# Visit places, two early banks, weights ahead of alpha and later query copies in a two-stage attention and MLP kernel

## The reference, cut to what matters

```
state = alpha[t][:, None] * state + outer(k[t], v[t])     # 4 batches, 8 heads, 768 tokens, 48 channels
y[t]  = q[t] @ state
x     = y, arranged as 3072 tokens x 384
h = x @ w_in  (384 x 2048);   g = h * sigmoid(1.702 h);   x = g @ w_out  (2048 x 384)
h = x @ w_in2 (384 x 2048);   g = h - tanh(h);            out = g @ w_out2 (2048 x 384)
```

## Time and profile before

| what | value |
|---|---|
| median of 3 executions | 976.02 us (975.45 to 976.64) |
| the profiled execution's own time | 975.9 us |
| its span | 974.1 us |
| TensorE busy | 951.4 us, 98% of the span |
| VectorE busy | 548.1 us, 56%, but 7 to 9 tenths in the first 18 of 40 slices |
| ScalarE / GpSimd busy | 334.1 us / 283.0 us |
| DMA | 59.07 MB; full in 26 to 40 us and in 44 to 50 us |

### The profile page before, as it was taken

How to read it: one execution, slowest core, us unless ns; L and a number is a source line. 1 busy time by engine, 2 the same in 40 slices (tenths; PEclk the granted TensorE clock), 3 DMA queues, 4 the chain that set the end, 5 groups by cost and what they waited for, 6 DMA issues and landing times.

```text
span 974.1 us, 22270 instructions
## 1 busy us (share of the span) xinstructions
PE 951.4 (98%) x9364; PEld 823.0 (84%) x9364; DVE 548.1 (56%) x1348; ACT 334.1 (34%) x683; POOL 283.0 (29%) x314
## 2 busy tenths in 40 slices
PE   5899999999999999999999999999999999999998
PEld 5789999999999988888888888888888888888886
DVE  7879997878888877776221223334334343343332
ACT  2342333332332332333234554333333333333332
POOL 2565655556556554444001542000000000000000
PEclk9999999999999999999999999999999999999999
DMA  7933232423323432321103332020020010200000
GB/s 156 262 82 88 56 86 48 112 51 80 84 61 62 115 64 47 103 50 22 36 38 126 96 96 74 0 65 1 1 66 1 24 41 1 65 1 1 33 1 33
DMA packets 136533, 59.07 MB, mean 61 GB/s; under 512 B 114288, under 2 KB 131824, under 8 KB 136432
## 3 DMA queue, kind: packets, MB, share of 16 engines
q1 hardware_dynamic: 133616, 55.54, 22.8%
q10 hardware_dynamic: 2816, 2.10, 0.7%
HBM read 43.45 MB, written 14.16 MB: 59 GB/s over the span
## 4 chain that ended last, share of the span: by engine, by line
PE 91%; DVE 3%; DMA 3%; SPq 1%; POOL 1%; issue 1%; ACT 1%; ACTq 0%; DVEq 0%; POOLq 0%
PE pX L760 38%; PE pZ L784 26%; PE pX L784 14%; PE pX L624 2%; PE pZ L719 2%; PE pZ L652 2%; PE pZ L610 1%; PE pZ L662 1%; DMA k<-k_t 1%; PE pX L755 1%; PE pX L638 1%; DVE scores L1065 1%; PE pZ L710 1%; SPq L323 1%; DVE w_lo L1071 1%; POOL r L518 1%
## 5 line engine op out<-in xcount | busy, mean ns | idle before, releaser
L760 PE MATMUL pX<-x_hi,w_hi 128*128 128x512 f32 (+2 forms) x624 | 227.9, 365 | 0.7 <-ACT g L913 0.7
L760 PE MATMUL pX<-x_hi,w_lo 128*128 128x512 f32 (+2 forms) x624 | 227.5, 365 | 0.0
L760 PE MATMUL pX<-x_lo,w_hi 128*128 128x512 f32 (+2 forms) x624 | 227.5, 365 | 0.0
L1081 DVE TENSOR_TENSOR g_lo<-g,g_hi 128x512 fp32r<-128x512 f32 (+2 forms) x208 | 133.3, 641 | 155.0 <-ACT g_hi L922 154.8
L1179 DVE TENSOR_TENSOR g<-pX,sg 128x512 f32<-128x512 f32 x96 | 66.3, 691 | 177.7 <-ACT sg L915 177.7
L784 PE MATMUL pZ<-g_hi,w_hi 128*128 128x512 f32 (+2 forms) x414 | 151.0, 365 | 0.0
L784 PE MATMUL pZ<-g_lo,w_hi 128*128 128x512 f32 (+2 forms) x414 | 150.9, 365 | 0.0
L784 PE MATMUL pZ<-g_hi,w_lo 128*128 128x512 f32 (+2 forms) x414 | 150.9, 364 | 0.0
L922 ACT ACTIVATE g_hi<-g 128x512 fp32r<-128x512 f32 (+2 forms) x208 | 121.3, 583 | 78.0 <-DVE g L1179 74.5
L913 ACT ACTIVATE g<-pX 128x512 f32<-128x512 f32 (+3 forms) x144 | 65.7, 456 | 212.6 <-PE pX L760 175.8
L760 PEld LDWEIGHTS pX<-x_hi,w_hi 128*128 128x128 f32 x624 | 117.6, 188 | 17.8 <-ACT g L913 1.1
(11 more groups left out here) (100 smaller groups left out, 1137.4 us busy)
## 6 DMA issues: line engine op xcount, KB each, us to landing
v<-v_l SPq DMA_DIRECT2D x96, 48.0 KB, 2.6
x_raw<-hidden SPq DMA_DIRECT2D x6, 768.0 KB, 5.8
attn_out<-y SPq DMA_DIRECT2D x94, 48.0 KB, 1.9
out_t<-o SPq DMA_DIRECT2D x10, 384.0 KB, 3.4
alpha<-a_t SPq DMA_DIRECT2D x24, 128.0 KB, 3.0
r<-q_t SPq DMA_DIRECT2D x24, 128.0 KB, 3.0
k<-k_t SPq DMA_DIRECT2D x24, 128.0 KB, 3.0
w_raw<-w_in SPq DMA_DIRECT2D x16, 192.0 KB, 2.4
```

The lines of the kernel that those rows point to most:

```text
L760: last = nc.tensor.matmul(pH(N)[:, 0:w], win(wp, f, m), XS[T % 2][xp][:, m, 0:w], start=(n == 0), stop=(n == len(terms) - 1))
L1081: nc.vector.tensor_tensor(GL[:, columns(N)], g_raw(N), GH[:, columns(N)].bitcast(F32), ALU.subtract).then_inc(gl_done, 1)
```

## The change

Four edits. The visits of items 3 to 16 move: item 3 from N = 4 to 6, 4 from 8 to 10, 5 from 12 to 14, 6 from 16 to 18, 7 from 20 to 22, 8 stays at 25, 9 goes from 30 to 32, 10 from 33 to 35, 11 from 36 to 38, 12 from 39 to 41, 13 from 42 to 44, 14 from 45 to 47, 15 from 49 to 50, 16 from 52 to 53; from item 17 (N = 55) on all are the same. up(1) and up(3) go into the bank O0 in place of H0, so that up(N) for N up to 4 waits for one activation less, while down(0) waits for the fourth activation and for the states of items 0 and 1. SP issues weight group 3 ahead of alpha of unit 3. The plain query copies stand one N later as long as the visit is in block 0 or 1 (with the moved visits: at N = 6, 14, 22, 31 in place of 3, 11, 19, 29, then 37 and 43 in place of 35 and 41, 49 in place of 48, and the same from there on). `x_at` is not changed.

```diff
-    starts = ([0, 4, 8, 12, 16, 20, 25, 30] + [33 + 3 * n for n in range(5)] + [49 + 3 * n for n in range(5)]
+    starts = ([0, 6, 10, 14, 18, 22, 25] + [32 + 3 * n for n in range(8)] + [55 + 3 * n for n in range(3)]
               + [64 + 2 * n for n in range(29)])
...
         def pH(N):
+            if N in (1, 3):
+                return O0
             return H0 if N < L1B * NF or N % 2 == 0 else H1
...
                 if U == 1:
                     load_w(sp, 2)
+                    load_w(sp, 3)
                 if U + 2 < UNITS:
                     load_alpha(U + 2)
-                if U == 1:
-                    load_w(sp, 3)
...
                 if N < L1N:
-                    if N:
-                        pe.wait_ge(g_done, N)
+                    if N > 1:
+                        pe.wait_ge(g_done, N if N > 4 else N - 1)
...
                 if T < PLAIN:
-                    pe.wait_ge(g_done, N + 1)
+                    pe.wait_ge(g_done, max(4, N + 1))
...
+                if N == 0:
+                    pe.wait_ge(state_step, states_before(LEAD))
                 for m in range(KC):
...
-            queries_at = {VISIT_OF[j + 1] - 1: j // 2 + 1 for j in range(LEAD, ITEMS - 2, 2)}
+            queries_at = {VISIT_OF[j + 1] - (VISIT_OF[j + 1] >= L1P): j // 2 + 1 for j in range(LEAD, ITEMS - 2, 2)}
...
-                    nc.scalar.activation(g_raw(N), H0[:, 0:width(T)], ACT.Gelu_apprx_sigmoid).then_inc(g_done, 1)
+                    nc.scalar.activation(g_raw(N), pH(N)[:, 0:width(T)], ACT.Gelu_apprx_sigmoid).then_inc(g_done, 1)
```

## The result

The changed kernel takes 985.43 us (median of 4, 984.14 to 986.89) against 975.74 us before: ratio 1.0092, 95% interval 1.0077 to 1.0107. It is slower by 9.7 us; I had forecast slower by 3.6. The profiled execution's span is 985.1 us against 974.1; at 986.9 us it is the slowest of the four.

A forecast was written before the change was run, and what follows sets the result against it. TensorE was taken as the bound, with VectorE's list setting block 2's earliest start. From 975.9 us: -1.1 balance from up(32), +1.7 low clock, +2.2 wait at block 3, +0.8 its clock = 979.5; range 975.8 to 982.2.

The forecast's parts named there:

- The step of block 3's input: At up(44): TensorE waits a new 2.2 us, since ScalarE's x_hi waits for the input load; bounds 1.2 and 3.
- Its clock: Low clock behind the wait at up(44): 0.8 us taken, bounds 0 and 1.7.
- The clock behind up(32): Low clock expected after 4.5 us of idle TensorE at up(32): 1.7 us, bounds 0 and twice that.
- Seven items in front of block 2: VectorE's list ahead of block 2 is unchanged, 29.1 us behind item 6's scores; x_lo ends at 92.7, bounds 91.3 and 95.
- The balance from up(32) on: 3.4 us gained by an earlier up(32), 2.83 given back for visit 9, 0.6 gained at visits 10 and 11: net gain 1.1.
- TensorE gains 2.5 us: Ahead of visit 3: early ups fit four more products (2.68 us) in for 0.14, so TensorE gains 2.5 us.
- The weights: Group 3 ahead of alpha of unit 3: alpha lands about 46.8 (bounds 43.0 and 49.5), so visit 5 waits 1.4 us.
- VectorE does not hold block 2: Faster rival: x_lo of block 2 could end at 86.7 in step with TensorE; 972.4 us, chance 0.13.
- the clock holds: No-change rival: the waits come without low clock; 977.0 us, or 975.8 with alpha landing as early as now; chance 0.15.
- The weights cost more: Slower rival: alpha of unit 3 at 49.5, x_lo at 94.5, both waits with full 1.7 us low clock; 982.2 us, chance 0.12.
- The copies still hold the keys: Rival: ScalarE's query copy of unit 3 still delays the keys; same time as the forecast, counted within its 0.60.
- The first rival: The case of x_lo of block 2 ending at 86.7 in step with TensorE; 972.4 us, chance 0.13.

The follow-up runs named there:

- v_visits: Kernel before with only the visits moved, plus the wait on the states of items 0 and 1 ahead of down(0); 985.1 us, ratio 1.0086.
- a_nobanks: Changed kernel without the early banks (up(1) and up(3) again into H0; the wait on the states stays); 985.84 us.
- a_noweights: Changed kernel with weight group 3 again issued behind alpha of unit 3; 985.46 us.
- a_xhigh44: Changed kernel with x_hi and x_lo of block 3 at N = 44 in place of 42; 980.4 us, ratio 1.0054 to the kernel before.
- v_late: Kernel before with only the later visits moved (item 9 at N = 32 and on every third slice, items 3 to 8 unmoved); 983.12 us, ratio 1.0078.
- a_fixed: Changed kernel with w_out remainders behind x_lo of block 2 and x_hi and x_lo of block 3 at N = 44; 973.45 us, ratio 0.9988.
- v_queries: Kernel before with only the later query copies; 974.35 us, ratio 0.9982.
- c_querieswlox13: Kernel before with later query copies, w_out remainders behind x_lo of block 2, and block 4's x_hi and x_lo at N = 61; 976.94 us, ratio 1.0020.
- v_banks: Kernel before with only the early banks (O0 for up(1) and up(3), with the waits that go with it); 974.48 us, ratio 0.9979.
- a_fixed_now: Changed kernel with late w_out remainders, block 3's x_hi and x_lo at N = 44, and weight group 3 again behind alpha; 974.19 us, ratio 0.9997.

## Why the prediction was wrong

**Direction and places right.** Slower, by the two waits I had named at up(32) and up(44), with the wait in visit 5 gone. The step of block 3's input had 2.2 us (bounds 1.2 and 3) and measured 2.4, with 2.9 between the visits; ScalarE waits for the input as described, behind the activation of slice 42:

```profile
139.26 0.84 ACT L876 ACTIVATE x_hi<-x_raw 128x768 fp32r<-128x768 f32 x1 [3.60 <-DMA x_raw<-attn_out]
```

Its clock, for which I took 0.8 between 0 and 1.7, is 1.0. The clock behind up(32) was put at 1.7 and is 1.9, by what is left over in the account above. That both terms come out so near is partly luck: the stretch behind up(32) is 6.8 us long and not 3.4 as in the trace that I took the price from, and the wait at up(44) is 3.1 to 3.4 us in v_visits, a_nobanks and a_noweights, above my bound of 3.

**What failed is the step "Seven items in front of block 2": the end of `x_lo`.** I took 92.7, with an upper bound of 95; it ended at 98.6, so up(32) came 5.9 us later than forecast, and the forecast misses by the same (979.5 against 985.4). The balance from up(32) on had 3.4 us gained from an `x_lo` earlier than before; there was no such gain, but 2.5 us of loss. VectorE in the changed kernel:

```profile
48.53 0.29 DVE L964 TENSOR_TENSOR sf<-alpha 112x128 f32<-112x128 f32 x1 [2.06 <-DMA alpha<-a_t]
...
66.85 0.42 DVE L1050 TENSOR_TENSOR scores<-pX,mask 128x256 f32<-128x256 f32 x1 [0.96 <-PE pX L639]
...
82.25 1.26 DVE L964 TENSOR_TENSOR t<-f 112x32 f32<-112x32 f32 x1
83.55 1.18 DVE L964 TENSOR_TENSOR f<-t 112x16 f32<-112x16 f32 x1
84.64 0.17 DVE L961 COPY f<-t 112x16 f32<-112x16 f32 x1
84.76 0.19 DVE L964 TENSOR_TENSOR f<-f,t 112x16 f32<-112x16 f32 x1
84.86 0.70 DVE L964 TENSOR_TENSOR t<-f 112x8 f32<-112x8 f32 x1
...
97.62 0.96 DVE L1080 TENSOR_TENSOR x_lo<-x_raw,x_hi 128x768 fp32r<-128x768 f32 x1
```

Two halves. First, item 6's scores started at 66.85 and not at 63.6, since TensorE was late: "TensorE gains 2.5 us" at visit 3 was wrong. I had costed the early ups by their waits alone. They ran 0.67 apart, and then TensorE stood still for 3.2 us with 3.4 us at a granted clock of 0.50 behind it, some 1.7 us of time; visit 3 began at 39.90 and not 35.1. Second, from item 6's scores to the end of `x_lo` are 31.7 us and not 29.1. The work is the same, as I said; the durations are not. The four product steps and the copy that took 0.17 to 0.19 us each before (80.54 to 81.17 for all) took from 82.25 to 85.48 here, 1.26, 1.18 and 0.70 for three of them. Visit 7 had moved from N = 20 to 22 and visit 8 stayed at 25, so visit 8 now begins 6.9 us behind it (9.6 before), and GpSimd's multiplications, which wait for visit 8's products, fall beside VectorE's steps for the next unit. Before, and then after:

```profile
80.54 0.19 DVE L961 TENSOR_TENSOR t<-f 112x32 f32<-112x32 f32 x1
80.77 0.19 DVE L961 TENSOR_TENSOR f<-t 112x16 f32<-112x16 f32 x1
```
```profile
82.15 1.31 POOL L534 TENSOR_TENSOR k<-k,sf 112x512 f32<-112x512 f32 x1 [2.15 <-PE pX L639]
83.42 5.56 POOL L519 TENSOR_TENSOR r<-r,alpha 112x512 f32<-112x512 f32 x5
```

Each of the three long steps starts about 0.1 us behind a GpSimd multiplication and ends within 0.05 us of that one's end (83.46, 84.68 and 85.53); the copy of the same size stays at 0.17, and one step, at 84.76, stays at 0.19. The Trainium skill, "SBUF — State Buffer", section "Who interferes with whom", says that VectorE and GpSimd share one pair of ports under an exclusive lock, and that a VectorE instruction with two SBUF inputs contends with a GpSimd instruction that reads SBUF. The trace agrees: three of the four operations with two inputs stretch and the copy does not. v_visits has the same pattern (1.31 and 1.22 us at 81 and 82 us) without the gap of 31 us. That the overlap is the cause is read from the traces; I did not move GpSimd's work to prove it.

Of the two, the second is what v_visits, a_nobanks, a_noweights and a_xhigh44 share with the changed kernel. In a_noweights item 6's scores start at 64.4, nearly where I had them, and `x_lo` still ends 31.1 us later, at 95.4. The gap is not shared: a_nobanks has none and is as slow. The size of the first half is also one of this execution: a_xhigh44, the same code up to block 3's input, has a gap of 0.8 us, waits 3.2 us for scores ahead of visit 5 instead, and ends `x_lo` at 100.5. Nor is the overlap the loss against the kernel before. `x_lo` ends at 95.4 to 96.8 in v_visits, a_nobanks and a_noweights and at 96.07 in the kernel before, and v_late, without long steps, is slow as well. What costs is that visit 9 was taken out of the very stretch in which TensorE then has nothing to do; I had set against it a gain at `x_lo` that did not come.

**The weights.** Alpha of unit 3 landed about 48.5, where I had 46.8 (bounds 43.0 and 49.5): it was issued at 41.13 and not 39.10, since GpSimd's first part had started 2 us later. The wait ahead of visit 5 did not come in this trace, because visit 5 was itself late; in a_fixed and a_xhigh44, whose gaps are short, it is there with 1.6 and 3.2 us (I had 1.4). The edit is neutral alone as well.

**The rivals.** "VectorE does not hold block 2" and "the clock holds" are refuted by the 6.7 us and the stretches at 0.50. "The weights cost more" had 982.2, near in size and wrong in its cause. "The copies still hold the keys" is refuted by v_queries. The first rival's time was also added up wrong: 6.5 + 0.6 gained less 2.2 and 0.8 from 975.9 gives 971.8 and not 972.4, which changes nothing here.

## What to carry to other kernels

Where one engine's list sets the start of a stage, work of the busy engine belongs in front of that start: the changed kernel waits 6.7 us in front of up(32) and makes visit 9, 2.8 us, behind it. When a block of work is moved, move with it every step that follows it at a fixed distance in another queue; here one table entry (input conversion at 44 in place of 42) and one list (16 remainders behind the stage's start) turn 985.4 into 973.5. And a sum of durations from a trace holds only while the same engines run side by side; ask what the move puts beside the list that binds.

## What the runs showed of the hardware

**TensorE seems to have run out of instructions.** The idle time at 31 us moves with the instruction stream, 12 records for 12. TensorE's two rows on the profile's page have 9364 instructions each, 18,728 together; queue 8, of kind instruction, has 74 packets of 16 KB, one for 253 of them. The packets fit the gap: in all twelve traces that have it at this place, TensorE goes on 2.5 to 3.0 us after the start of a packet of queue 8. In the changed kernel, v_late and c_querieswlox13, with the gaps of 3.2, 1.6 and 1.9 us, that packet starts at 31.8, 31.7 and 32.3; in the kernel before and in v_banks it starts at 29.5, and the kernel before, slower to get there, has no gap. The Trainium skill, "Runtime: NRT & Kernel Launch", section "Instruction fetch mechanics", says that an engine's instructions are refilled in blocks of 16 KiB, which are 256 instructions, and calls the cost mostly hidden. Here it is not always: while data transfers keep the 16 DMA engines busy (DMA share 0.8 to 1.2 from 24 to 48 us), TensorE stands still for 0.7 to 3.2 us in all ten kernels with early banks, as it gets to the place sooner, and for 1.6 and 1.9 us in two with one bank; v_visits has a gap of 1.1 us elsewhere, at 47 us. That queue 8 feeds TensorE is read from these counts and times, and that the busy DMA engines delay the packet was not tested.

**The clock after a wait.** With 6.7 us of idle went 6.8 us at 0.50, the first 1.7 of them still inside the wait; 2.4 us among full products left 3.4; 2.2 in visit 5 before left 3.4; 1.3 and 1.4 at up(32) left none. The length of the wait does not settle it: 3.2 us at up(32) in a_fixed_now left none, 3.4 us at up(44) in a_noweights left 6.8, and in c_querieswlox13 a gap of 1.9 us left 6.8. In the changed kernel the stretches behind up(32) and up(44) cost 1.9 and 1.0 us beyond the waits.
